# Windowed attention in a fused kernel: groups of 64 queries with two heads block-diagonal, in place of tiles of 128 queries per head

## What is computed

```python
# attention: q, k, v are (2, 8, 768, 64); block 32, window 16
k_sum = k.reshape(B, H, nb, 32, D).max(axis=3)
v_sum = v.reshape(B, H, nb, 32, D).mean(axis=3)
scores_l = scale * q @ k.T, kept where |pos_q - pos_k| < 16, else -1e9
scores_s = scale * q @ k_sum.T + log(32)
a = softmax(concat([scores_l, scores_s]));  attn = a @ concat([v, v_sum])
# first block: x is attn with the heads side by side, (2, 768, 512)
gate = sigmoid(causal_conv5(x, conv_w));  y = (gate * (x @ w_val)) @ w_out
# second block
h = relu(y @ w_in);  u, v = halves of h;  v_n = layer_norm(v)
out = (u * (w_spatial @ v_n + b_spatial)) @ w_out2
```

## Time and profile before

| | |
|---|---|
| median of 3 runs | 330.44 us (327.86 to 331.41) |
| profiled execution, its own time | 328.2 us |
| its span, first to last instruction | 326.4 us |
| PE busy | 311.4 us (95%) |
| DVE busy | 200.2 us (61%) |
| ACT busy | 145.8 us (45%) |
| POOL busy | 118.7 us (36%) |
| DMA | 49465 packets, 25.33 MB, of the packets 43914 under 512 B |
| granted TensorE clock | 1.00 throughout |

### The profile page before, as it was taken

The page is one execution under the profiler, slowest core; times in us unless marked ns, Lnnn a source line. Parts: engine busy times, 40 slices in busy tenths (PEclk is TensorE's granted clock), DMA queues, the critical chain, the costliest instruction groups (busy, mean ns, idle before and its releaser), DMA issues.

```text
span 326.4 us, 5515 instructions
## 1 busy us (share of the span) xinstructions
PE 311.4 (95%) x1876; PEld 289.1 (89%) x1876; DVE 200.2 (61%) x605; ACT 145.8 (45%) x423; POOL 118.7 (36%) x135
## 2 busy tenths in 40 slices
PE   7689999999999999869999999999999999999996
PEld 6569999999998999767889999888899999998886
DVE  5999999999989999998420000687865432420000
ACT  3279888878996453233322222443342111122112
POOL 7007258479433487524200000143449433230000
PEclk9999999999999999999999999999999999999999
DMA  8886896897351053300000000121101000002222
GB/s 188 161 187 133 163 229 155 190 195 182 90 148 51 2 177 83 96 1 0 3 0 0 2 0 0 50 67 62 35 32 32 2 0 0 2 0 96 98 96 96
DMA packets 49465, 25.33 MB, mean 78 GB/s; under 512 B 43914, under 2 KB 44190, under 8 KB 49054
## 3 DMA queue, kind: packets, MB, share of 16 engines
q1 hardware_dynamic: 49438, 24.99, 30.9%
HBM read 21.24 MB, written 3.15 MB: 75 GB/s over the span
## 4 chain that ended last, share of the span: by engine, by line
PE 53%; DVE 0%; ACT 0%; issue 0%
PE psum L632 51%; PE psum L716 1%; DVE work L1051 0%; ACT work L868 0%
## 5 line engine op out<-in xcount | busy, mean ns | idle before, releaser
L480 POOL TENSOR_TENSOR g_lo<-work,g_hi 128x384 fp32r<-128x384 f32 x32 | 32.3, 1025 | 40.2 <-ACT g_hi L861 26.1
L766 ACT ACTIVATE probs<-neg_s,neg_max 128x184 f32<-128x184 f32 x96 | 42.1, 441 | 10.0 <-DVE neg_max L881 9.7
L480 POOL TENSOR_TENSOR vn_lo<-work,vn_hi 128x512 fp32r<-128x512 f32 x12 | 15.5, 1295 | 72.4 <-DVE vn_hi L1088 72.4
L569 PE MATMUL psum<-k_win,qT 128*128 128x184 f32 x192 | 38.5, 323 | 2.8 <-DVE neg_max L881 1.4
L569 PEld LDWEIGHTS psum<-k_win,qT 128*128 128x128 f32 x192 | 29.5, 191 | 4.0 <-issue 2.2
L881 DVE CUSTOM_DVE_ANT_0 neg_s<-psum,mask 128x184 f32<-128x184 f32 x96 | 31.0, 343 | 1.5 <-PE psum L569 1.2
L1066 DVE TENSOR_TENSOR wsp_lo<-psum,wsp_hi 128x384 fp32r<-128x384 f32 x12 | 6.6, 548 | 33.3 <-ACT wsp_hi L842 33.3
L780 ACT ACTIVATE probsT<-psum 128x384 f32<-128x384 f32 x48 | 23.2, 484 | 8.1 <-PE psum L578 7.8
L901 DVE TENSOR_TENSOR probs<-probs,psum 128x368 f32<-128x368 f32 x48 | 25.6, 533 | 0.9
L1098 DVE TENSOR_TENSOR work<-psum,b_row 128x384 f32<-128x384 f32 x16 | 8.9, 558 | 28.1 <-PE psum L632 26.5
L962 DVE SCALAR_TENSOR_TENSOR psum<-xT,conv_c,psum 128x384 f32<-128x384 f32 x48 | 26.1, 613 | 0.0
(11 more groups left out here) (125 smaller groups left out, 758.7 us busy)
## 6 DMA issues: line engine op xcount, KB each, us to landing
k_nat<-in_k_dram SPq DMA_DIRECT2D x16, 192.0 KB, 3.4
q_nat<-in_q_dram SPq DMA_DIRECT2D x16, 192.0 KB, 3.6
v_blk<-in_v_dram SPq DMA_DIRECT2D x4, 768.0 KB, 6.8
v_main<-in_v_dram SPq DMA_DIRECT2D x16, 192.0 KB
out_dram<-work SPq DMA_DIRECT2D x11, 256.0 KB, 2.0
raw<-in_moe_w_spatial_dram SPq DMA_DIRECT2D x6, 384.0 KB, 3.2
raw<-in_moe_w_out_dram SPq DMA_DIRECT2D x8, 256.0 KB, 2.8
raw<-in_moe_w_in_dram SPq DMA_DIRECT2D x8, 256.0 KB, 3.1
```

What stands on the lines that cost most here:

```text
L480: nc.gpsimd.tensor_tensor(dst_lo, src, dst_hi.bitcast(F32), ALU.subtract).then_inc(lo_sem, 1)
L569: ins = nc.tensor.matmul(bank_s(i, h), qT[:, s, h, t * P:(t + 1) * P], k_win[:, s, t, KEYS[h]], start=True, stop=True)
L766: ins = nc.scalar.activation(probs[:, i % RING, w], neg_s[:, i % 3, w], ACT.Exp, bias=neg_max[:, i % 4, h:h + 1], scale=-1.0, accum_out=su ...
```

## The change

Queries go in groups of 64. The stationary operand of a score product is now a block-diagonal 128x128 tile: the first head's 64 queries in partitions 0 to 63 and columns 0 to 63, the second's in the other halves. Both heads share one range of 120 keys per group: 64 own, 16 before, 16 after, 24 summaries, one below the other in `k_win` (the heads lie in different partitions). A step is still 128 queries of two heads, now two groups g. Per step there are two score products of 120 columns, two transposes in place of three, two value products in place of three, each on its own with `v_win` (120 rows, both heads side by side). Of each value product the two diagonal blocks are wanted, so the output is taken in two copies of 64 partitions, one by ACT, one by DVE (`take_x` on both). V is loaded straight into `v_win`: 96 rows of each inner group, so that neighbouring groups read 32 rows twice; the means are copied to 12 groups in place of 6 tiles.

With it: `sum_k` leaves DVE, its copy becomes a third one in `k_tails` on POOL; the means of the first v_blk go to POOL (`mean_v(0)`, ahead of `k_tails(1)`); the zeros of `qT` are written by DVE; the three masks are made by POOL alone; Q has two buffers and is loaded two pairs ahead; V of pair 0 is loaded before the loop, V of later pairs behind K and Q of pair p+2; `w_out` pieces are loaded later (PIECES_OF); 20 in place of 10 convolution instructions stand in the drain of the attention; 4 in place of 12 warming transposes before the first scores.

```diff
-    SIDE = 2 * WINDOW + NB
-    HEAD, SC, WIDE = P + SIDE, 2 * (P + SIDE), P + 2 * SIDE
-    MAIN, LEFT, RIGHT, SUMS = SIDE, 0, WINDOW, 2 * WINDOW
-    KEYS = (slice(MAIN, WIDE), slice(0, HEAD))
-    MAIN_A, REST, MAIN_B = 0, P, P + 2 * SIDE
+    GROUP = P // 2
+    GROUPS = S // GROUP
+    NEAR = GROUP + 2 * WINDOW
+    KEYS = NEAR + NB
+    assert KEYS <= P and NEAR % BLOCK == 0
...
-            q_nat = sb("q_nat", [P, 1, T, P], F32, att)
+            q_nat = sb("q_nat", [P, 2, T, P], F32, att)
             k_nat = sb("k_nat", [P, 2, T, P], F32, att)
-            qT = sb("qT", [P, 2, 2, S], F32, att)
-            probsT = sb("probsT", [P, 2, 3 * P], F32, att)
+            qT = sb("qT", [P, 2, GROUPS, P], F32, att)
...
-                k_win = sb("k_win", [P, 2, T, WIDE], F32, att)
+                k_win = sb("k_win", [P, 2, GROUPS, KEYS], F32, att)
                 k_max = sb("k_max", [P, NB], F32, att)
-                v_rest = sb("v_rest", [P, 2, T, 2 * D], F32, att)
+                v_win = sb("v_win", [P, 2, GROUPS, P], F32, att)
...
+        def keys_at(p, piece):
+            n = PIECE // GROUP
+            return k_win[:, p % 2, n * piece:n * (piece + 1), WINDOW:WINDOW + GROUP]
+        def by_group(x):
+            return x.rearrange("p (g n) -> p g n", n=GROUP)
+        def bank_s(i):
+            return psum[:, i % 2, 0:2 * KEYS].rearrange("p (g n) -> p g n", n=KEYS)
+        bank_t = psum[0:KEYS, 2, 0:2 * P].rearrange("p (g n) -> p g n", n=P)
...
-                    x = v_h[2 * p + h].rearrange("(t r) d -> r t d", r=P)
-                    d, row = slice(h * D, (h + 1) * D), h * SIDE
-                    sp.dma_start(v_main[:, s, :, 2 * h * D:(2 * h + 1) * D], x).then_inc(done, 16)
-                    sp.dma_start(v_rest[row + LEFT:row + LEFT + WINDOW, s, 1:T, d],
-                                 x[P - WINDOW:P, 0:T - 1, :]).then_inc(done, 16)
-                    sp.dma_start(v_rest[row + RIGHT:row + RIGHT + WINDOW, s, 0:T - 1, d],
-                                 x[0:WINDOW, 1:T, :]).then_inc(done, 16)
+                    x, d = v_h[2 * p + h], slice(h * D, (h + 1) * D)
+                    near = x[GROUP - WINDOW:GROUP - WINDOW + NEAR, :]
+                    near = bass.AP(near.tensor, near.offset, [[D, NEAR], [GROUP * D, GROUPS - 2], [1, D]])
+                    sp.dma_start(v_win[0:NEAR, s, 1:GROUPS - 1, d], near).then_inc(done, 16)
+                    sp.dma_start(v_win[WINDOW:NEAR, s, 0, d], x[0:NEAR - WINDOW, :]).then_inc(done, 16)
+                    sp.dma_start(v_win[0:NEAR - WINDOW, s, GROUPS - 1, d],
+                                 x[S - NEAR + WINDOW:S, :]).then_inc(done, 16)
+            def load_means(p):
+                s, done = p % 2, v_loaded[p % 2]
                 sp.wait_ge(v_mean_ready, p // 2 + 1)
-                for h, row in enumerate((SUMS, SIDE + SUMS)):
+                for h in range(2):
                     n = (2 * (p % 2) + h) * NB
                     src = v_mean[n:n + NB, (p // 2) % 2, :]
-                    src = src.rearrange("n (a d) -> n a d", a=1).broadcast_to((NB, T, D))
-                    sp.dma_start(v_rest[row:row + NB, s, :, h * D:(h + 1) * D], src).then_inc(done, 16)
+                    src = src.rearrange("n (a d) -> n a d", a=1).broadcast_to((NB, GROUPS, D))
+                    sp.dma_start(v_win[NEAR:KEYS, s, :, h * D:(h + 1) * D], src).then_inc(done, 16)
...
+            load_heads(1, q_h, q_nat, q_loaded, q_turned)
+            load_v(0)
             for p in range(PAIRS):
-                if p + 1 < PAIRS:
-                    load_heads(p + 1, q_h, q_nat, q_loaded, q_turned)
-                load_v(p)
                 if p + 2 < PAIRS:
                     load_heads(p + 2, k_h, k_nat, k_loaded, k_turned)
+                    load_heads(p + 2, q_h, q_nat, q_loaded, q_turned)
+                if p >= 1:
+                    load_v(p)
+                load_means(p)
...
+                nc.gpsimd.tensor_copy(k_win[:, s, 1:GROUPS, 0:WINDOW], k_win[:, s, 0:GROUPS - 1, GROUP:GROUP + WINDOW])
+                nc.gpsimd.tensor_copy(k_win[:, s, 0:GROUPS - 1, NEAR - WINDOW:NEAR],
+                                      k_win[:, s, 1:GROUPS, WINDOW:2 * WINDOW])
+                pool.wait_ge(k_max_ready, PIECES * (p + 1))
+                nc.gpsimd.tensor_copy(k_win[:, s, :, NEAR:KEYS], k_max[:, :].rearrange(
+                    "p (a n) -> p a n", a=1).broadcast_to((P, GROUPS, NB))).then_inc(k_tails_ready, 1)
...
-            nc.gpsimd.memset(qT[:, 0, :, :], 0.0).then_inc(q_zeros, 1)
+            nc.gpsimd.memset(k_win[:, :, 0, 0:WINDOW], 0.0)
+            nc.gpsimd.memset(k_win[:, :, GROUPS - 1, NEAR - WINDOW:NEAR], 0.0).then_inc(pool_zeros, 1)
             make_mask()
-            nc.gpsimd.memset(qT[:, 1, :, :], 0.0).then_inc(q_zeros, 1)
             k_tails(0)
+            mean_v(0)
...
-                for h in range(2):
-                    ins = nc.tensor.matmul(bank_s(i, h), qT[:, s, h, t * P:(t + 1) * P], k_win[:, s, t, KEYS[h]],
+                for g in range(2):
+                    ins = nc.tensor.matmul(bank_s(i)[:, g, :], qT[:, s, 2 * t + g, :], k_win[:, s, 2 * t + g, :],
                                            start=True, stop=True)
...
-                for n, first in enumerate((MAIN_A, MAIN_B, REST)):
-                    ins = nc.tensor.transpose(bank_t[:, n * P:(n + 1) * P], probs[:, i % RING, first:first + P],
-                                              ident[:, :])
+                for g in range(2):
+                    ins = nc.tensor.transpose(bank_t[:, g, :], probs[:, i % RING, g, :], ident[:, :])
...
-                    pe.wait_ge(xT_ready, i // 2 - 1)
-                o = bank_x(i)[:, i % 2 * P:i % 2 * P + P]
-                pT = probsT[:, i % 2, :]
-                nc.tensor.matmul(o, v_main[:, s, t, 0:P], pT[:, 0:P], start=True, stop=False)
-                nc.tensor.matmul(o, v_main[:, s, t, D:D + P], pT[:, P:2 * P], start=False, stop=False)
-                nc.tensor.matmul(o, v_rest[:, s, t, :], pT[:, 2 * P:3 * P], start=False,
-                                 stop=True).then_inc(x_summed, 1)
+                    wait_x(pe, i - 2)
+                for g in range(2):
+                    ins = nc.tensor.matmul(bank_x(i)[:, i % 2 * 2 + g, :], v_win[0:KEYS, s, 2 * t + g, :],
+                                           probsT[0:KEYS, i % 2, g, :], start=True, stop=True)
+                ins.then_inc(x_summed, 1)
...
-                nc.scalar.activation(x_of(p, r * P, 2 * P), bank_x(2 * j)[:, 0:2 * P],
-                                     ACT.Copy).then_inc(xT_ready, 1)
+                nc.scalar.activation(by_group(x_of(p, r * P, 2 * P)[0:D]), bank_x(2 * j)[0:D, :, 0:GROUP],
+                                     ACT.Copy).then_inc(xA_ready, 1)
...
+            def take_x(j):
+                dve.wait_ge(x_summed, 2 * j + 2)
+                p, r = divmod(2 * j, T)
+                nc.vector.tensor_copy(by_group(x_of(p, r * P, 2 * P)[D:P]),
+                                      bank_x(2 * j)[D:P, :, GROUP:P]).then_inc(xB_ready, 1)
...
-            def sum_k(p):
-                dve.wait_ge(k_max_ready, PIECES * (p + 1))
-                if p >= 2:
-                    dve.wait_ge(scores_ready, T * (p - 1))
-                sums_of = k_max[:, :].rearrange("p (a n) -> p a n", a=1)
-                ins = nc.vector.tensor_copy(sides(p, 0, T, SUMS, NB), twice(sums_of.broadcast_to((P, T, NB))))
-                ins.then_inc(k_sum_ready, 1)
...
-            nc.vector.memset(v_rest[:, :, :, :], 0.0).then_inc(v_zeros, 1)
-            nc.vector.memset(v_main[:, :, :, D:2 * D], 0.0).then_inc(v_zeros, 1)
+            for n, rows_of in ((0, slice(0, 2 * WINDOW)), (GROUPS - 1, slice(GROUP, NEAR))):
+                nc.vector.memset(v_win[rows_of, :, n, :], 0.0).then_inc(v_zeros, 1)
             nc.vector.memset(sums[:, :, :, 1:2], 1e-9).then_inc(eps_set, 1)
             nc.vector.memset(xT[:, :, 0:PAD], 0.0).then_inc(x_zeros, 1)
-            dve.wait_ge(mask_step, MASK_STEPS)
-            for e in (0, 2):
-                nc.vector.tensor_copy(mask[:, e, :], mask[:, 1, :]).then_inc(edge_step, 1)
-            dve.wait_ge(edge_step, 2)
-            for n in (0, HEAD):
-                nc.vector.memset(mask[:, 0, n + LEFT:n + LEFT + WINDOW], OUTSIDE)
-                ins = nc.vector.memset(mask[:, 2, n + RIGHT:n + RIGHT + WINDOW], OUTSIDE)
-            ins.then_inc(edge_step, 1)
-            dve.wait_ge(edge_step, 3)
+            for s in range(2):
+                nc.vector.memset(qT[:, s, :, :], 0.0).then_inc(q_zeros, 1)
...
-            for i in range(STEPS + 4):
+            for i in range(STEPS + 8):
                 p, t = divmod(i, T)
-                if i >= 4:
+                if 4 <= i < STEPS + 4:
                     normalise(i - 4)
-                if i == 0:
-                    add_blocks(0)
-                if i == 1:
-                    for level in range(1, LEVELS):
-                        add_blocks(level)
```

(17 more changed lines are left out.)

127 lines of the change are left out of this document (51 added, 76 removed).

## The result

The changed kernel takes 332.99 us (median of 20 runs, 330.61 to 337.86), the kernel before on the same chip 330.34 (20 runs, 327.86 to 331.92). The ratio is 1.0065, 95% interval 1.0043 to 1.0087: 0.7% slower, where 325.4 us and 1.5% faster were forecast, with a range of 317 to 331.

A forecast was written before the change was run, and what follows sets the result against it. The prediction took attention as bound by DVE and PE almost equally, DVE after the change, and the convolution by DVE alone. Terms -5.9 - 1.0 - 0.2 + 2.1 = -5.0 us from the 330.44 us median gave 325.4 us, range 317 to 331.

The forecast's parts named there:

- The gain up to step 12: Start of the kernel: first mask 2.9 us earlier, mostly lost in a wait at step 12; gain 1.0 us, ends 3.9 and -1.
- the sum: Whole kernel: all terms together -5.0 us on the profiled execution of 328.2 us, giving 323.2 us.
- five pairs, -5.9 us: Steps 12 to 42: DVE still binds at 10.19 us a pair, 50.95 us in place of 56.83.
- had room: Transfers during attention: 170 GB/s went with a share of 0.79 of the engines' time, so more would fit.
- have some 3 us to spare: Attention pairs: the v_blk loads later than the second were said to have some 3 us of slack.
- the transfers become the bound (slower): Attention pairs: at no more than 170 GB/s a pair needs 11.9 us, the kernel takes 334.0 us; chance 0.10.
- The last pair, -0.2 us: Steps 42 to 48: PE waits about 2 us for w_out, DVE about 1.2; gain 0.2 us, ends 1.3 and -1.5.
- a way to be wrong: Attention: the granted clock, 1.00 all through, might fall now that PE is busy 78% of a step.
- The drain, +2.1 us: Behind the last pair: four more take_x 1.8, normalisations -0.5, DVE's wait for g_lo 0.8; loss 2.1 us, ends 0.5 and 3.5.
- Swallowed: Whole kernel: dearer take_x, low start and worse last pair eat the gain; 331.5 us at most, 329 middle; chance 0.18.
- PE alone as the bound: Attention pairs: they follow PE, 15 us less, and the time is near 311 us; chance 0.05.
- three quarters of 0.50 with 0.17 and 0.05: Chance of faster, given as 0.61: part of own sum's 0.50, cheap take_x with open start 0.17, PE alone 0.05.

The follow-up runs named there:

- the execution profiled first: The changed kernel unaltered, in the longest of its 20 runs, against a median of 332.99 us; 337.86 us.
- experiment 9: Changed kernel with weight pieces loaded as in the kernel before and the large V transfer cut to one row from pair 2 on; 327.33 us, ratio 0.9915.
- experiment 12: Changed kernel with weight pieces loaded as before and without the second to fourth v_blk and their means on POOL; 325.86 us, ratio 0.9865.
- experiment 10: Changed kernel with SP's order of the transfers as in the kernel before, Q keeping its second buffer; 331.99 us, ratio 1.0085.
- experiment 3: Changed kernel with the large V transfer cut to one row of each group from pair 2 on; 330.62 us, ratio 1.0022.
- 8: Changed kernel with every transpose of K and Q made twice, more work for PE; 331.87 us, ratio 1.0057.
- experiment 17: Changed kernel, take_x on ACT, pieces as before, V and means ahead of K and Q, third v_blk ahead of V, fourth behind means; 325.21 us, ratio 0.9847.
- experiment 5: Changed kernel with the weight pieces loaded behind the same pairs as in the kernel before; 331.52 us, ratio 1.0008.
- experiment 2: Changed kernel with Q of pair 1, and V of pair 0 behind it, issued only when Q of pair 0 is turned; 332.43 us, ratio 1.0059.
- 1: The changed kernel as it is, run and profiled again; 334.44 us, ratio 1.0135 to the kernel before.
- 6: Changed kernel with means of the second to fourth V block behind the next even pair's key copies on POOL; 332.19 us, ratio 0.998.
- 11: Changed kernel with each later v_blk issued ahead of V and means of its pair; 333.87 us, ratio 1.014.
- experiment 13: Changed kernel with DVE's half of take_x given to ACT for the last four copies, in the drain, alone; median 328.89 us, 0.997.

## Why the prediction was wrong

**The costs of single instructions were right.** PE's step 1.32 (forecast 1.33), `take_x` 0.46 (0.46), a pair without waits 10.27 to 10.28 (10.19), step 12 at 32.66 (33); the first mask stood at 10.08 us, and at 9.59 in the execution profiled first (9.5). PE waits for DVE in the steady steps, as forecast. The gain up to step 12 was 0.95 us, forecast 1.0. With v_blk out of the way the whole came to 323.59 us, 0.4 from the sum, but that nearness is partly luck: against the kernel before, the stretches of that execution differ by -1.26 up to step 12, -5.27 in five pairs, -1.24 in the last and +3.17 in the drain, and the medians by 4.1 us, where the forecast had 5.0.

**The step that failed first: five pairs, -5.9 us.** Measured -2.82. It took the content for the time, since the transfers "had room": the share of 0.79 of the earlier trace rows and the 21 ns a packet of the earlier trace rows gave 7.8 us for the small packets of a pair. That counts an average over pairs. What it left out are data that come at a time of their own. The sentence that later v_blk "have some 3 us to spare" stands beside a forecast that opens step 36 at 73.4 us (33.61 - 1.0 + 4 x 10.19), 6.4 ahead of the kernel before. The fourth v_blk and the keys behind it did not come 6.4 us earlier in the changed kernel, nor earlier at all. In the kernel before:

```profile
68.54 5.46 POOL L458 TENSOR_TENSOR v_blk<-v_blk 96x1024 f32<-96x1024 f32 x5 [2.15 <-DMA v_blk<-in_v_dram]
...
74.78 0.32 POOL L446 COPY k_win<-k_win 128x160 f32<-128x160 f32 x1
...
79.73 0.54 DVE L901 TENSOR_TENSOR probs<-probs,psum 128x368 f32<-128x368 f32 x1
```

In the changed kernel, whose step 36 opens at 76.08, right behind them, and in experiment 9, where most of V is not loaded from pair 2 on:

```profile
68.98 5.44 POOL L469 TENSOR_TENSOR v_blk<-v_blk 96x1024 f32<-96x1024 f32 x5 [3.39 <-DMA v_blk<-in_v_dram]
...
75.48 0.43 POOL L456 COPY k_win<-k_max 128x288 f32<-128x288 f32 x1
```

```profile
68.16 5.44 POOL L470 TENSOR_TENSOR v_blk<-v_blk 96x1024 f32<-96x1024 f32 x5 [1.40 <-DMA v_blk<-in_v_dram]
...
74.66 0.43 POOL L457 COPY k_win<-k_max 128x288 f32<-128x288 f32 x1
```

Without the later v_blk (12) step 36 opens at 73.63, where the forecast had it. The rival "the transfers become the bound (slower)", with a chance of 0.10, was nearest to this, but neither its rate nor its place was right: it took a steady 170 GB/s, and they moved 199 from 34 to 60, with a share of 1.00; and PE did not wait for V of a pair, but for K, the means, `k_win` behind v_blk and `w_out` in turn. Nor does the share decide: from 34 to 88 us it is 0.64 in experiment 9, with a pair of 13.74 us, and 0.97 in experiment 10, with none over 11.01.

What did fill up is SP. In the changed kernel it is inside an issue for 65.2 of the 68 us from 12 to 80, before for 55.5, in experiment 9 for 64.7 (fewer bytes, as many transfers), in experiment 12 for 53.0. The difference is mostly in Q of two pairs later, issued behind v_blk and K, which holds SP over 4 us each time (last section); the median time from issue to landing rose from 3.4 to 5.2 us for K and from 3.6 to 6.1 for Q. That this sets when the later v_blk and the means go out is what the traces suggest; no experiment took issues away and left the rest.

**The last pair, -0.2 us, was +3.19.** The wait for the third piece of `w_out` was forecast at 2 us for PE and came to 2.81, but its price on DVE at 1.2, and that was 3.85 and 0.70. Between the two stands the clock: it fell to 0.50 for 6 us behind the wait. The forecast gave the clock as a way to be wrong and named the wrong trigger, the 78% busy steps. Those ran at 1.00 in the stretches free of long waits (from 45 to 88 us in experiment 3, from 34 to 88 in experiment 12), and a busier PE gained nothing (8). In the changed kernel it fell behind waits of 2.50, 2.80 and 2.81 us, but also from 54 to 58 us, behind two of 0.73 and 1.17 us close together; waits of 2.63 us for Q in experiment 10 and of 2.77 for K in experiment 17 left it at 1.00. So no single length divides them. For this one place, the wait for `w_out`, all profiles in which DVE takes its half of the output agree: behind 1.1, 1.45, 1.59 and 1.99 us (9, 5, 10, 2) the clock stayed at 1.00 and the pair took 10.2 to 11.1 us, behind 2.23 to 3.09 us (1, 3, 6, 8, 11, 13 and the execution of 337.86 us) it fell and the pair took 13.0 to 14.3. At the forecast's 2 us the forecast's pair of 10.7 would have been nearly right: 11.13 in experiment 2.

**The drain, +2.1 us, was +3.12,** within its ends 0.5 and 3.5. `take_x` costs its 1.8 and one wait more for POOL's `g_lo`, 1.31 us where it was 0.37. The forecast charged 2.1 for this and bought -5.9 with the rest; experiment 13 says that four copies of 24 were nearly the whole cost of `take_x`, because in the pairs DVE waits for data anyway (with all of them on ACT the five pairs take 55.03 us).

**Swallowed** had the right size of gain up to step 48 (1.0 us by its terms, 0.6 measured) and the wrong reasons (`take_x` at 0.57). Two figures of the prediction don't follow from its own terms, without bearing on the result: PE alone as the bound gives 316 us with its 15 us, not 311, and three quarters of 0.50 with 0.17 and 0.05 is 0.60, not 0.61.

Open: what weighs most at step 36, the bytes of v_blk, its issue behind a full SP, or POOL's 6 us of sums. Experiment 9 (fewer bytes of V, same chain) left 13.74 us there, experiment 12 (no v_blk, no sums) 10.28; the sums without the bytes, and fewer issues with the same bytes, weren't tried. Why a single execution of the same kernel can differ by 7 us isn't shown either; with the waits hanging on transfers, small shifts in these may decide.

## What to carry to other kernels

When the engine that binds gets faster, read from the trace of before how late each transfer and each helper's result could have come, and subtract the new lead from every one of them at its own place; a mean DMA share below 1 says nothing of when one load lands. Look also at how long the engine that issues the transfers is held by them. Price a wait of PE at what it costs after it as well, as long as the clock may be at its lower level behind it. And put an added copy where the engine that takes it waits anyway, not in the drain where it alone sets the end.

## What the runs showed of the hardware

- Behind a wait of PE of 2.81 us the granted clock was 0.50 for 6 us (93 to 99), behind one of 3.20 us (experiment 5) 0.50 from 78 to 84; behind one of 1.45 (5), one of 2.63 (10) and one of 2.77 us (17) it stayed at 1.00. Before the change the start had a wait of 2.39 us without a fall.
- A DMA issue on SP is held up when transfers queue. In the changed kernel two Q transfers of 192 KB took SP 1.13 us to issue at 1.81 us, and 4.45 us later on, behind v_blk, a weight piece and two K transfers (of the second one alone the issue took 3.80 us):

```profile
62.54 0.54 SPq L375 DMA_DIRECT2D v_blk<-in_v_dram  x1
63.12 0.42 SPq L387 DMA_DIRECT2D raw<-in_moe_w_val_dram  x1
63.58 1.23 SPq L345 DMA_DIRECT2D k_nat<-in_k_dram  x2
64.88 4.45 SPq L345 DMA_DIRECT2D q_nat<-in_q_dram  x2
```

Everything that SP issues after that, V and the means of the next pair here, goes out later. In experiment 12, without the later v_blk, no such pair of issues between 12 and 87 us took over 2 us. A forecast that places issues by the waits in the program alone has them too early.
